# A loop of three turns in place of TensorE's unrolled attention steps, with one transpose added at two waits of each step

## The chip, the core and the metric

The kernel runs on one core of a Trainium2 chip. The metric is the device time of one execution in microseconds, lower is better; a median of several executions is given. Besides it there is a profile of one execution: for every engine the instructions with their start and duration. The engines are TensorE (PE in the profile; its weight loads are PEld, and what its sequencer does alone is PEldq), VectorE (DVE), ScalarE (ACT), GpSimd (POOL) and SyncE (SP), which here only issues the DMA transfers.

## What is computed

Attention over 2 x 8 heads, 576 positions and 64 channels, in two parts that are added; then a SiLU block and four weighted ReLU blocks over 1152 tokens of 512 channels.

```python
q_d = q.reshape(B, H, Sd, factor, D).mean(axis=3)      # factor 4; k_d and v_d likewise
out_up = np.repeat(sm_attn(q_d, k_d, v_d), factor, axis=2)
mask = np.abs(pos[:, None] - pos[None, :]) < factor
scores = np.where(mask, scale * q @ k.T, -1e9)
out_local = softmax(scores) @ v
x = (out_up + out_local), heads side by side           # 1152 x 512
h = x @ w_in;  x = (h * sigmoid(h)) @ w_out            # w_in 512 x 2048
out = sum over e of p[:, e] * (relu(x @ w1[e]) @ w2[e])   # 4 times 512 x 1024
```

## The kernel before

Every engine has a program of its own, written out by hand, and they meet at semaphores alone. There are N = 8 pairs of heads, and the attention is a pipeline over them. On TensorE step s does, in this order:

- scores(s): the mask as two matmuls against the identity, and 36 small score matmuls on top of it (lines 698 and 705 of the profile). They need the loaded q and k of pair s, and the bank back, which the normalised probabilities pl of pair s-1 tell.
- scores_down(s): four matmuls for the downsampled attention (line 718).
- turn_p0(s-1): four transposes of pl (line 659).
- values(s-2): 36 small matmuls with the transposed probabilities and a window of v (line 732), and the downsampled ones (line 739).
- turn_p1(s-1): the last transpose of pl and eight small ones of the downsampled probabilities pd (lines 659 and 664).

Each matmul in float32 is two matmuls and two weight loads in the profile, except transposes, which are one of each. So a step has 177 matmuls and 177 weight loads.

Meanwhile VectorE and ScalarE do the softmax of pair s in turn: VectorE the maximum and the subtraction, ScalarE the exponential, VectorE sum, reciprocal and product (line 559, which writes pl). ScalarE also copies what turn_p0(s-1) put into PSUM, and does so ahead of the exponential of pair s. GpSimd adds neighbouring positions for the downsampling, computes the low halves of x and of the first weight units. SyncE issues the loads of pair s+1 and the window of v for pair s-1.

Ahead of step 2 TensorE runs warm-up transposes of the identity in five groups (WARM; line 656): 12 ahead of all, 4 and 12 in step 0, 8 in step 1 between scores_down(1) and turn_p0(0), 5 ahead of scores(2). The steps are a Python loop, so TensorE's program has all of them one after another. In the last steps the first two tiles of layer one, in1(0, 0) and in1(0, 1) (line 753), are put between the transposes and values(7). From there on TensorE works through layer one and the four blocks of layer two (lines 753, 794, 810), in which it has hardware loops already: layer one's token blocks 1 and 2 are a loop of two turns (line 839), each with 16 tiles of 12 matmuls in and 12 out.

Of the kernel before, what the change touches and what calls it, by code (L numbers as in the profile page):

```python
# [14 lines left out]
P = 128  # L15
# [10 lines left out]
def program(nc, qk, vw, vr, w, probs, out, dims):  # L26
# [3 lines left out]
    SD = S // R  # L30
    HQ = SD // 2
# [26 lines left out]
    with ExitStack() as ctx:  # L58
# [3 lines left out]
        def sem(name):  # L62
            return ctx.enter_context(nc.semaphore(name))
# [9 lines left out]
        def asb(name, shape):  # L73
            return sb(name, shape, F32, att)
# [10 lines left out]
        ident = asb("ident", [P, P])  # L85
# [281 lines left out]
        def _(act):  # L367
            def copy(dst, src):
                return act.activation(dst, src, ACT.Copy)  # L369
# [52 lines left out]

            def evac_up(n):
                act.wait_ge(pv_done, n + 1)
                if n >= 1:
                    act.wait_ge(xf_done, n)
                copy(up[:, :].rearrange("p (a i q) -> p a i q", a=2, q=GQ // R),
                     ps[:, OUTB + 1, HC:HC + SD].rearrange("p (i a q) -> p a i q", a=2, q=GQ // R)).then_inc(up_done, 1)

            def x_high(n):  # L430
                act.wait_ge(xf_done, n + 1)
                copy(x_of(x_hi, n), xf[:, n, :]).then_inc(xhi_done, 1)

            def step(s):
# [71 lines left out]
        def _(dve):  # L506
            dve.memset(ident[:, :], 0.0).then_inc(zeroed, 1)
            dve.memset(band[:, :], 0.0).then_inc(zeroed, 1)
            dve.memset(pl[:, :, :, 0, W:HS], 0.0).then_inc(zeroed, 1)
            DSTEPS = 4  # L510

            def own(n, k):
                return n * DSTEPS + k

# [123 lines left out]
            with dve.Fori(0, E) as e:  # L638
                with dve.Fori(0, BLOCKS) as blk:
                    for f in range(FT2):  # L640
                        hidden2(e * (BLOCKS * FT2) + blk * FT2 + f, f)
                    for j in range(TT):
                        n = e * (BLOCKS * TT) + blk * TT + j
# [6 lines left out]
                            in1=o, op0=ALU.mult, op1=ALU.add).then_inc(out_done, 1)  # L650

        @block.tensor
        def _(pe):
            def warm(count):
                for _ in range(count):
                    pe.transpose(ps[:, OUTB, 0:P], ident[:, :], ident[:, :])  # L656

            def turn_local(n, bank, at, t):
                return pe.transpose(ps[0:PW, TB + bank, at:at + P],  # L659
                                    pl[:, n % 2, t, :, :].rearrange("p h j -> p (h j)")[:, 0:PW], ident[:, :])  # L660

            def turn_down(n, bank, at, i):
                s, h, half = i // 4, (i // 2) % 2, i % 2
                return pe.transpose(ps[0:HQ, TB + bank, at:at + HQ],  # L664
                                    pd[:, n % 2, 2 * h + half, s * HQ:(s + 1) * HQ], ident[0:HQ, 0:HQ])

            def turn_p0(n):
                pe.wait_ge(pl_ready, n + 1)
                if n == 0:
                    pe.wait_ge(zeroed, 3)  # L670
                if n >= 1:
                    pe.wait_ge(pd_out, n)
                for t in range(GT - 1):
                    ins = turn_local(n, 0, t * P, t)
                ins.then_inc(p0_turned, 1)

            def turn_p1(n):
                if n >= 1:
                    pe.wait_ge(p1_out, n)
                turn_local(n, 1, 0, GT - 1)  # L680
                pe.wait_ge(pd_ready, n + 1)
                for i in range(5):
                    ins = turn_down(n, 1, P + i * HQ, i)
                ins.then_inc(p1_turned, 1)
                pe.wait_ge(p0_out, n + 1)
                for i in range(3):
                    ins = turn_down(n, 0, i * HQ, 5 + i)
                ins.then_inc(pd_turned, 1)

            def scores(n):  # L690
                par = n % 2
                pe.wait_ge(qk_in[par], 16 * (n // 2 + 1))
                if n >= 1:
                    pe.wait_ge(pl_ready, n)
                else:
                    pe.wait_ge(mask_set, QP + 2)
                for h in range(2):
                    pe.matmul(ps[:, SLB + h, 0:LC], ident[:, :], mask[:, :, :].rearrange("p t j -> p (t j)"),  # L698
                              start=True, stop=False, skip_group_check=True)
                for g in range(G):  # L700
                    t, c = g // QP, g % QP
                    at = t * W
                    for h in range(2):
                        rows = slice(D * h, D * h + D)
                        ins = pe.matmul(ps[GQ * c:GQ * c + GQ, SLB + (h ^ g % 2), at:at + W],  # L705
                                        qk_raw[rows, par, GQ * g:GQ * g + GQ],
                                        qk_raw[rows, par, S + GQ * g:S + GQ * g + W], start=False, stop=True,
                                        skip_group_check=True)
                ins.then_inc(s_full, 1)

            def scores_down(n):
                pe.wait_ge(qkd_ready, 2 * n + 2)
                if n >= 1:
                    pe.wait_ge(pd_ready, n)
                for half in range(2):
                    for h in range(2):
                        rows = slice(D * h, D * h + D)
                        ins = pe.matmul(ps[0:HQ, SDB + h, half * SD:half * SD + SD],  # L718
                                        qd[rows, half * HQ:half * HQ + HQ], kd[rows, :], start=True, stop=True)
                ins.then_inc(sd_full, 1)  # L720

            def values(n):
                par = n % 2
                pe.wait_ge(p0_out, n + 1)
                pe.wait_ge(p1_out, n + 1)
                pe.wait_ge(vw_in[par], 32 * (n // 2 + 1))
                if n >= 1:
# [14 lines left out]
                ins.then_inc(pv_done, 1)  # L742
# [19 lines left out]
            def step(s):  # L762
                if s == N + 1:
                    in1(0, 1)
                if s == 2:
                    warm(WARM[4])
                stage(s, scores)
                if s == 0:
                    warm(WARM[1])
                stage(s, scores_down)  # L770
                if s < 2:
                    warm(WARM[2 + s])
                stage(s - 1, turn_p0)
                stage(s - 2, values)
                if s == N:
                    pe.wait_ge(xlo_done, XHALF)
                    pe.wait_ge(pd_ready, N)
                    in1(0, 0)
                stage(s - 1, turn_p1)
# [49 lines left out]
            pe.wait_ge(pl_ready, N)  # L829
            pe.wait_ge(pd_out, N)  # L830
            out1(0, 0)
            pe.wait_ge(xf_done, N)
            in1(0, 2)
            for f in range(3, FT1 + 2):
                if f < FT1:
# [49 lines left out]
```

## Time and profile before

| | |
|---|---|
| median of 3 executions | 680.59 us (678.07 to 682.2) |
| the profiled execution | 682.4 us, of it 680.5 from the first to the last instruction |
| TensorE busy | 665.4 us (98%), 4625 matmuls |
| VectorE, ScalarE, GpSimd busy | 156.5, 182.9, 164.6 us |
| instruction transfers of queue 8 | 21, 0.34 MB |
| mean granted TensorE clock | 0.976 of 2.4 GHz |

Busy TensorE means that a matmul is under way, at whatever clock. The clock that was granted is given as a share of 2.4 GHz: 1.00 is 2.4 GHz, 0.50 is 1.2. In the chain of waits "issue" is time in which the engine waited for nothing that the profile shows. Times in the rows are microseconds from the start of the span, those called mean, median or duration of one instruction nanoseconds.

### The profile page before, as it was taken

What the parts mean: (1) busy time and instruction counts of PE and PEld (TensorE: products, weight loads), DVE (VectorE), ACT (ScalarE), POOL (GpSimd) and SP (SyncE); (2) the same over time, 40 slices, a digit from 0 to 9 for tenths busy, and PEclk for the clock granted to TensorE, in tenths of its full rate; (3) what the DMA queues carried; (4) which work ended last, traced back from release to release, by engine and by line L of the source; (5) the groups of instructions that cost most, each with busy time, mean ns of one, the idle gap of its engine ahead of it and who ended that gap; (6) DMA issues with size and microseconds to landing.
All of it is one profiled execution on the core that took longest, in us unless ns stands there. A gap on an engine that the chain in (4) does not pass through costs nothing.

```text
span 680.5 us, 11829 instructions
## 1 busy us (share of the span) xinstructions
PE 665.4 (98%) x4625; PEld 616.8 (91%) x4625; DVE 156.5 (23%) x291; ACT 182.9 (27%) x385; POOL 164.6 (24%) x127
## 2 busy tenths in 40 slices
PE   7898999999999999999999999999999999999997
PEld 6676999999999999999898989898989898989996
DVE  5665311121112111212121212121212212121211
ACT  3555554332223244441111331010331010111010
POOL 4777476500000045561000460000550000000000
PEclk9786899999999999999999999999999999999999
DMA  8776124200000013331000140000220000000101
GB/s 262 180 196 142 59 110 153 95 1 1 1 0 1 0 67 124 118 129 57 0 0 0 63 155 31 0 0 0 92 92 0 0 0 0 0 31 16 46 0 46
DMA packets 11228, 38.59 MB, mean 57 GB/s; under 512 B 1536, under 2 KB 1536, under 8 KB 11200
## 3 DMA queue, kind: packets, MB, share of 16 engines
q1 hardware_dynamic: 11200, 38.19, 17.6%
q8 instruction: 21, 0.34, 0.2%
q14 instruction: 7, 0.06, 0.0%
HBM read 35.83 MB, written 2.36 MB: 56 GB/s over the span
## 4 chain that ended last, share of the span: by engine, by line
PE 97%; issue 1%; DVE 1%; ACT 0%; DVEq 0%; POOL 0%; POOLq 0%
PE ps L753 45%; PE ps L810 29%; PE ps L794 15%; PE ps L732 2%; PE ps L698 1%; PE ps L659 1%; PE ps L705 1%; PE ps L718 1%; PE ps L739 1%; PE ps L664 1%; PE ps L656 1%; DVE pl L559 0%; DVE ps L550 0%; DVE o_acc L647 0%; ACT plT L369 0%
## 5 line engine op out<-in xcount | busy, mean ns | idle before, releaser
L465 ACT ACTIVATE g_hi<-ps 128x384 fp32r<-128x384 f32 x96 | 47.2, 492 | 301.7 <-PE ps L753 301.7
L618 DVE SCALAR_TENSOR_TENSOR g_lo<-ps,g_hi 128x384 fp32r<-128x384 f32 x96 | 53.5, 557 | 270.5 <-ACT g_hi L465 270.5
L321 POOL TENSOR_TENSOR wa_lo<-w_raw,wa_hi 128x1024 f32 x20 | 47.9, 2401 | 215.4 <-ACT wa_hi L369 215.3
L753 PE MATMUL ps<-x_hi,wa_hi 128*128 (+1 forms) x288 | 97.6, 339 | 0.0
L753 PE MATMUL ps<-x_hi,wa_lo 128*128 (+1 forms) x288 | 97.4, 338 | 0.0
L753 PE MATMUL ps<-x_lo,wa_hi 128*128 (+1 forms) x288 | 97.2, 338 | 0.0
L753 PE MATMUL ps<-x_hi,wb_hi 128*128 (+1 forms) x288 | 96.9, 336 | 0.0
L753 PE MATMUL ps<-x_lo,wb_hi 128*128 (+1 forms) x288 | 96.9, 336 | 0.0
L753 PE MATMUL ps<-x_hi,wb_lo 128*128 (+1 forms) x288 | 96.8, 336 | 0.0
L321 POOL TENSOR_TENSOR wb_lo<-w_raw,wb_hi 128x1024 f32 x24 | 57.5, 2403 | 103.3 <-ACT wb_hi L369 103.0
L596 DVE TENSOR_TENSOR g_lo<-ps,g_hi 128x384 fp32r<-128x384 f32 x48 | 26.8, 557 | 155.1 <-ACT ps L460 155.1
L810 PE MATMUL ps<-wa_hi,g_lo 128*128 128x512 f32 x144 | 56.7, 394 | 0.0
L810 PE MATMUL ps<-wb_hi,g_lo 128*128 128x512 f32 x144 | 56.7, 394 | 0.0
L810 PE MATMUL ps<-wa_lo,g_hi 128*128 128x512 f32 x144 | 56.7, 394 | 0.0
L753 PEld LDWEIGHTS ps<-x_hi,wa_hi 128*128 128x128 f32 x288 | 54.6, 190 | 1.9 <-issue 0.4
L810 PE MATMUL ps<-wb_lo,g_hi 128*128 128x512 f32 x144 | 56.4, 391 | 0.0
L810 PE MATMUL ps<-wb_hi,g_hi 128*128 128x512 f32 x144 | 56.3, 391 | 0.0
L753 PEld LDWEIGHTS ps<-x_lo,wa_hi 128*128 128x128 f32 x288 | 54.6, 190 | 1.5
L810 PE MATMUL ps<-wa_hi,g_hi 128*128 128x512 f32 x144 | 56.0, 389 | 0.0
L753 PEld LDWEIGHTS ps<-x_lo,wb_hi 128*128 128x128 f32 x288 | 54.0, 188 | 1.6
L753 PEld LDWEIGHTS ps<-x_hi,wb_hi 128*128 128x128 f32 x288 | 54.0, 188 | 1.4
L753 PEld LDWEIGHTS ps<-x_hi,wa_lo 128*128 128x128 f32 x288 | 54.6, 190 | 0.0
(96 smaller groups left out, 923.5 us busy)
## 6 DMA issues: line engine op xcount, KB each, us to landing
w_raw<-w SPq DMA_DIRECT2D x48, 512.0 KB, 3.4
qk_raw<-qk SPq DMA_DIRECT2D x8, 579.0 KB, 5.9
v_win<-vw SPq DMA_DIRECT2D x16, 216.0 KB, 5.1
v_raw<-vr SPq DMA_DIRECT2D x8, 288.0 KB
out<-o_acc SPq DMA_DIRECT2D x9, 256.0 KB, 2.0
pr<-probs SPq DMA_DIRECT2D x1, 18.0 KB, 6.6
```

Of the source, the lines that this page charges most:

```text
L321: pool.tensor_tensor(lo[:, at, :].rearrange("p o n -> p (o n)"), w_raw[:, s, :], hi[:, at, :].rearrange("p o n -> p (o n)").bitcast(F32), ...
L465: act.activation(g_hi[:, f % GB, :], ps[:, HB + f % 4, 0:NB], ACT.Relu).then_inc(relu_done, 1)
L596: dve.tensor_tensor(g_lo[:, f % GB, :], ps[:, HB + f % 4, 0:NB], g_hi[:, f % GB, :].bitcast(F32), ALU.subtract).then_inc(g_ready, 1)
L618: dve.scalar_tensor_tensor(out=g_lo[:, f % GB, :], in0=ps[:, HB + f % 4, 0:NB], scalar=0.0, in1=g_hi[:, f % GB, :].bitcast(F32), op0=ALU.m ...
L656: pe.transpose(ps[:, OUTB, 0:P], ident[:, :], ident[:, :])
L659: return pe.transpose(ps[0:PW, TB + bank, at:at + P], pl[:, n % 2, t, :, :].rearrange("p h j -> p (h j)")[:, 0:PW], ident[:, :])
L664: return pe.transpose(ps[0:HQ, TB + bank, at:at + HQ], pd[:, n % 2, 2 * h + half, s * HQ:(s + 1) * HQ], ident[0:HQ, 0:HQ])
L698: pe.matmul(ps[:, SLB + h, 0:LC], ident[:, :], mask[:, :, :].rearrange("p t j -> p (t j)"), start=True, stop=False, skip_group_check=True)
L732: pe.matmul(ps[D * h:D * h + D, OUTB + g % 2, at:at + GQ], v_win[p0:p0 + W, par, g, :], plT[p0:p0 + W, par, t, GQ * c:GQ * c + GQ], start= ...
L753: ins = pe.matmul(dst, w[:, f % HALF, c], x[:, kt, at], start=(kt == 0 and i == 0), stop=(kt == KT - 1 and i == 2))
L794: ins = pe.matmul(ps[:, ACCB + j, 0:NB], w[:, f % HALF, c], g[:, f % GB, :], start=(f == 0 and i == 0), stop=(f == FT1 - 1 and i == 2))
L810: ins = pe.matmul(ps[:, ACCB + j, 0:DM], g[:, f % GB, c], w[:, f % HALF, KT * P:UNIT], start=(f == 0 and i == 0), stop=(f == FT2 - 1 and i ...
```

## The change

TensorE's steps 0 and 1 and what follows step 7 are written out; steps 2 to 7 become a loop (`pe.Fori`) of three turns over two steps. All addresses stay constants, since the two buffers alternate within a turn; the thresholds of the waits are computed from the loop's register. scores_down gets a transpose of the identity behind its waits, into columns of its own bank that nobody reads, and so does values. So that values(0) needs no case of its own, xf_done starts at one: VectorE sets a column of up to zero and raises it, and all waits on xf_done ask for one more. The eight warm-up transposes of step 1 come behind turn_p0(0), not ahead of it.

```diff
@@ scalar
             def evac_up(n):
                 act.wait_ge(pv_done, n + 1)
-                if n >= 1:
-                    act.wait_ge(xf_done, n)
+                act.wait_ge(xf_done, n + 1)
@@ vector
+            dve.memset(up[:, 0:1], 0.0).then_inc(xf_done, 1)
@@ tensor
-            def turn_p0(n):
+            def turn_p0(n, par):
                 pe.wait_ge(pl_ready, n + 1)
-                if n == 0:
+                if par == 0 and isinstance(n, int) and n == 0:
                     pe.wait_ge(zeroed, 3)
-                if n >= 1:
+                else:
                     pe.wait_ge(pd_out, n)
-            def scores(n):
-                par = n % 2
-                pe.wait_ge(qk_in[par], 16 * (n // 2 + 1))
-                if n >= 1:
+            def scores(n, par, turn):
+                pe.wait_ge(qk_in[par], 16 * turn + 16)
+                if not (isinstance(n, int) and n == 0):
                     pe.wait_ge(pl_ready, n)
             def scores_down(n):
-                pe.wait_ge(qkd_ready, 2 * n + 2)
-                if n >= 1:
+                pe.wait_ge(qkd_ready, n * 2 + 2)
+                if not (isinstance(n, int) and n == 0):
                     pe.wait_ge(pd_ready, n)
+                pe.transpose(ps[:, SDB + 1, 3 * SD - P:3 * SD], ident[:, :], ident[:, :])
-            def values(n):
-                par = n % 2
+            def values(n, par, turn):
                 pe.wait_ge(p0_out, n + 1)
                 pe.wait_ge(p1_out, n + 1)
-                pe.wait_ge(vw_in[par], 32 * (n // 2 + 1))
-                if n >= 1:
-                    pe.wait_ge(xf_done, n)
+                pe.wait_ge(vw_in[par], 32 * turn + 32)
+                pe.wait_ge(xf_done, n + 1)
+                pe.transpose(ps[:, OUTB, HC:HC + P], ident[:, :], ident[:, :])
-            for s in range(N + 2):
-                step(s)
+            scores(0, 0, 0)
+            warm(WARM[1])
+            scores_down(0)
+            warm(WARM[2])
+            scores(1, 1, 0)
+            scores_down(1)
+            turn_p0(0, 0)
+            warm(WARM[3])
+            turn_p1(0, 0)
+            warm(WARM[4])
+            with pe.Fori(1, N // 2) as i:
+                for par in range(2):
+                    s = i * 2 + par
+                    scores(s, par, i)
+                    scores_down(s)
+                    turn_p0(s - 1, 1 - par)
+                    values(s - 2, par, i - 1)
+                    turn_p1(s - 1, 1 - par)
+            turn_p0(N - 1, 1)
+            values(N - 2, 0, N // 2 - 1)
+            pe.wait_ge(xlo_done, XHALF)
+            pe.wait_ge(pd_ready, N)
+            in1(0, 0)
+            turn_p1(N - 1, 1)
+            in1(0, 1)
+            values(N - 1, 1, N // 2 - 1)
```

## Rows read from the trace of the kernel before

**Rows 1.** The chain that ended last: its shares of the span by engine
```profile
PE 97%; issue 1%; DVE 1%; ACT 0%; DVEq 0%; POOL 0%; POOLq 0%
```

**Rows 2.** The same chain in order of time: start us, us, what
```profile
24.50 2.37 issue
...
38.99 0.49 issue
...
49.53 0.47 issue
...
53.91 2.33 issue
```

**Rows 3.** Stretches: window us, PE busy (instructions), granted clock, DMA share, GB/s
```profile
27.10:37.30 10.20, 10.20 (x186) 0.50 0.78 183
...
40.70:44.10 3.40, 3.40 (x87) 0.50 0.47 123
44.10:57.80 13.70, 10.68 (x338) 1.00 0.66 164
57.80:74.80 17.00, 16.31 (x242) 0.50 0.44 102
```

**Rows 4.** One stretch, of PE, PEld, DVE, ACT, POOL busy (instructions), clock, DMA
```profile
26.87:38.99 12.12, 12.11 (x251) 9.61 (x251) 6.92 (x15) 5.21 (x19) 7.84 (x12) 0.58 0.81 204
```

**Rows 5.** DMA queues from 139 to 206.4 us (first row), from 206.4 to 273.5 (others)
```profile
q8 instruction: 4, 0.07, 0.4%
...
q1 hardware_dynamic: 1000, 3.65, 14.7%
q14 instruction: 1, 0.01, 0.0%
```

**Rows 6.** The second turn of layer one's loop, columns as in rows 4
```profile
206.40:273.50 67.10, 67.10 (x385) 67.10 (x385) 11.06 (x20) 25.16 (x44) 17.68 (x8) 1.00 0.15 55
```

**Rows 7.** Step 1: two rows of the chain, one of the timeline
```profile
12.79 1.02 PE ps L656 x8
...
14.78 0.49 ACT ps L409
...
12.77 0.56 DVE L536 TENSOR_TENSOR ps<-ps,mx 128x380 f32<-128x380 f32 x1
```

**Rows 8.** The chain at the low clock: four transposes of 128 columns
```profile
59.39 1.02 PE ps L659 x4
```

**Rows 9.** TensorE's sequencer by line: duration ns min/median/max, first and last start us
```profile
L747 PEldq EVENT_SEMAPHORE  x88: 51/51/51, 68.3 to 664.3; - x88
L747 PEldq ALU_OP  x42: 32/32/32, 141.2 to 647.7; - x42
L747 PEldq FUSED_REGOPS  x14: 42/125/136, 139.2 to 639.5; - x14
...
L839 PEldq COMPARE_BRANCH  x2: 76/159/242, 206.4 to 273.6; - x2
```

**Rows 10.** The chain: where scores of steps 5 to 7 and turn_p0(7) start
```profile
41.70 1.36 PE ps L698 x4
...
48.13 0.88 PE ps L698 x4
...
56.69 0.69 PE ps L698 x4
...
65.69 1.06 PE ps L659 x4
```

**Rows 11.** The chain: values(6) and values(7)
```profile
66.75 2.08 PE ps L732 x72
...
77.28 1.18 PE ps L732 x72
```

**Rows 12.** A stretch as in rows 4; the loads of v_win, from issue to landing
```profile
50.00:60.00 10.00, 7.66 (x218) 6.14 (x217) 6.62 (x14) 4.12 (x16) 9.69 (x13) 0.89 0.70 168
...
DMA to landing us min/median/max: 3.3/5.1/7.8
```

More of the change, by code:

```diff
@@ L430, in x_high @@
             def x_high(n):
-                act.wait_ge(xf_done, n + 1)
+                act.wait_ge(xf_done, n + 2)
                 copy(x_of(x_hi, n), xf[:, n, :]).then_inc(xhi_done, 1)
@@ L656, in warm, with turn_local, turn_down, turn_p1 @@
                     pe.transpose(ps[:, OUTB, 0:P], ident[:, :], ident[:, :])
-            def turn_local(n, bank, at, t):
+            def turn_local(par, bank, at, t):
                 return pe.transpose(ps[0:PW, TB + bank, at:at + P],
-                                    pl[:, n % 2, t, :, :].rearrange("p h j -> p (h j)")[:, 0:PW], ident[:, :])
-            def turn_down(n, bank, at, i):
+                                    pl[:, par, t, :, :].rearrange("p h j -> p (h j)")[:, 0:PW], ident[:, :])
+            def turn_down(par, bank, at, i):
                 s, h, half = i // 4, (i // 2) % 2, i % 2
                 return pe.transpose(ps[0:HQ, TB + bank, at:at + HQ],
-                                    pd[:, n % 2, 2 * h + half, s * HQ:(s + 1) * HQ], ident[0:HQ, 0:HQ])
-            def turn_p0(n):
+                                    pd[:, par, 2 * h + half, s * HQ:(s + 1) * HQ], ident[0:HQ, 0:HQ])
+            def turn_p0(n, par):
                 pe.wait_ge(pl_ready, n + 1)
-                if n == 0:
+                if par == 0 and isinstance(n, int) and n == 0:
                     pe.wait_ge(zeroed, 3)
-                if n >= 1:
+                else:
                     pe.wait_ge(pd_out, n)
                 for t in range(GT - 1):
-                    ins = turn_local(n, 0, t * P, t)
+                    ins = turn_local(par, 0, t * P, t)
                 ins.then_inc(p0_turned, 1)
-            def turn_p1(n):
-                if n >= 1:
+            def turn_p1(n, par):
+                if not (isinstance(n, int) and n == 0):
                     pe.wait_ge(p1_out, n)
-                turn_local(n, 1, 0, GT - 1)
+                turn_local(par, 1, 0, GT - 1)
                 pe.wait_ge(pd_ready, n + 1)
                 for i in range(5):
-                    ins = turn_down(n, 1, P + i * HQ, i)
+                    ins = turn_down(par, 1, P + i * HQ, i)
                 ins.then_inc(p1_turned, 1)
@@ L686, in turn_p1 @@
                 for i in range(3):
-                    ins = turn_down(n, 0, i * HQ, 5 + i)
+                    ins = turn_down(par, 0, i * HQ, 5 + i)
                 ins.then_inc(pd_turned, 1)
-            def scores(n):
-                par = n % 2
-                pe.wait_ge(qk_in[par], 16 * (n // 2 + 1))
-                if n >= 1:
+            def scores(n, par, turn):
+                pe.wait_ge(qk_in[par], 16 * turn + 16)
+                if not (isinstance(n, int) and n == 0):
                     pe.wait_ge(pl_ready, n)
@@ L711, in scores_down @@
             def scores_down(n):
-                pe.wait_ge(qkd_ready, 2 * n + 2)
-                if n >= 1:
+                pe.wait_ge(qkd_ready, n * 2 + 2)
+                if not (isinstance(n, int) and n == 0):
                     pe.wait_ge(pd_ready, n)
+                pe.transpose(ps[:, SDB + 1, 3 * SD - P:3 * SD], ident[:, :], ident[:, :])
                 for half in range(2):
@@ L720, in scores_down @@
                 ins.then_inc(sd_full, 1)
-            def values(n):
-                par = n % 2
+            def values(n, par, turn):
                 pe.wait_ge(p0_out, n + 1)
                 pe.wait_ge(p1_out, n + 1)
-                pe.wait_ge(vw_in[par], 32 * (n // 2 + 1))
-                if n >= 1:
-                    pe.wait_ge(xf_done, n)
+                pe.wait_ge(vw_in[par], 32 * turn + 32)
+                pe.wait_ge(xf_done, n + 1)
+                pe.transpose(ps[:, OUTB, HC:HC + P], ident[:, :], ident[:, :])
                 for g in range(G):
@@ L760, in _ @@
             WARM = (12, 4, 12, 8, 5)
[L762 to L779, printed above, removed]
             pe.wait_ge(ident_set, 1)
             warm(WARM[0])
-            for s in range(N + 2):
-                step(s)
+            scores(0, 0, 0)
[24 more added lines that the diff above has]
+            values(N - 1, 1, N // 2 - 1)
             def layer_out1(t, blk, f, w_hi, w_lo):
@@ L831, in _ @@
             out1(0, 0)
-            pe.wait_ge(xf_done, N)
+            pe.wait_ge(xf_done, N + 1)
             in1(0, 2)
```

## The prediction

> **What bounds the kernel now.** I read four views in this order. First the chain that ended last: 97% of it is TensorE work [rows 1], so what counts is where TensorE waits or runs slowly. Second, the same chain in order of time. After 79 us it has no wait in it worth naming; all that can be won lies in the attention steps ahead of that. There are four waits there that nothing in the profile releases ("issue"): 2.37, 0.49, 0.47 and 2.33 us [rows 2] (a fifth, shorter one lies in step 2). Third, the granted clock by stretch: it is at the low level (1.2 GHz) from 27.1 to 37.3, from 40.7 to 44.1 and from 57.8 to 74.8 us, and at the high one (2.4 GHz) between [rows 3]. Each fall comes within 4 us after one of the "issue" waits: 26.87 is followed by 27.1, 39.48 by 40.7, 56.24 by 57.8. The fifth wait, of 0.47 us at 49.53, and the softmax waits around 48 us did not bring the clock down.
>
> What are those waits? Between the end of the first at 26.87 and the start of the second at 38.99 TensorE executed 251 matmuls and 251 weight loads [rows 4]. With the sequencer's ten separate waits between them that is twice 256, and the other distances come out as once or twice 256 in the same way: the waits lie on a grid of 256 instructions. Instruction transfers of queue 8 are about 0.07 MB for 4, near 16 KB each, or 64 bytes an instruction [rows 5]. I take the waits for code that came late. Not every border costs something; those do which fall on a stretch with full data queues.
>
> **What a loop does to that.** The six looped steps hold eight such borders; as three turns over two steps only the first turn has to load code, if the blocks stay. The kernel before has a loop of this very size: layer one's loop over token blocks runs 385 matmuls and 385 loads a turn, as its second turn shows [rows 6]. An attention step has 177 matmuls and 177 loads, so a turn of two has 358 of each with the added transposes, slightly less. In the first turn of layer one's loop queue 8 fetched 4 blocks; in the second the transfers were those of queue 1 and one of queue 14, none of queue 8 [rows 5]. So a taken branch back over 770 instructions found its code in place.
>
> The Trainium skill says otherwise (Runtime: NRT & Kernel Launch, section Instruction fetch mechanics): only two blocks of 16 KB are kept, and a taken branch to a target outside them forces a fetch. By that rule each turn here would load again and the sum would be the second rival's, not mine. The rows of layer one's loop speak against it; but there long matmuls were queued over the branch, and at the end of an attention turn only short ones are, so the rule keeps a chance.
>
> **The sum**, against the profiled execution (span 680.5 us, 682.4 us in all; the median of the runs is 680.59, so this execution is 1.8 us slow). Everything is reckoned to the end of the last attention matmuls at about 79 us; after it TensorE is continuous, so what is won there is won at the end.
>
> 1. *Ahead of step 2.* The eight warm-up transposes of step 1 (1.02 us [rows 7]) move from ahead of turn_p0(0) to behind it. They stood on the path: turn_p0, its copy on ScalarE, then the exponential at 14.78 [rows 7]. Next late would be VectorE's subtraction, over at 13.33 [rows 7]. Gain 0.9 (bounds 0.5 and 1.02). Two added transposes, 0.13 us each (1.02/8), lie on the path: +0.26. Net -0.6.
> 2. *The other 14 transposes.* At the high clock 0.13 us [rows 7]; at the low one 0.26, by four 128-column transposes in 1.02 us [rows 8]. Step 2: 0.26. Steps 3 and 4, mostly low: 0.9. Steps 5 to 7: the one in scores_down delays turn_p0, its copy and the exponential, so 0.13 each; the one in values stands where TensorE has about 0.2 us to spare, I charge half. 0.6 in all. values(6) and values(7): 0.26. Sum +2.0 (bounds 0.9, if only those in scores_down count at the high clock, and 3.6, all 14 at the low price).
> 3. *Waits against registers.* A step has 15 waits in the Python code, whose thresholds are computed now. Known prices on TensorE's sequencer: 32 ns for an addition, 42 to 136 for a fused one, 51 for a separate wait [rows 9]; the step before had about six separate waits, 0.3 us. All 15 exposed at 51 ns would be 0.77; if they only replace the six, nothing or 0.3 less. Queued behind them are small matmuls, 72 of which pass in 1.18 us, 16 ns each [rows 11], so little work covers them as it does in layer one, except where TensorE waits for softmax anyhow. I take +0.15 a step, nearest to the 32 ns row with a third hidden: +0.9 for six (bounds -0.3 and +2.8).
> 4. *Back edges.* 242 ns at most for a taken branch, 76 for one not taken [rows 9]; two taken with a register move after each: +0.6.
> 5. *Late code in steps 4 to 7.* 0.49 + 0.47 + 2.33 = -3.3. The waits of steps 2 and 3 (a short one and 2.37) stay: that is the first turn, with the data queues as full as before (bounds: -5.7 if the 2.37 goes too, 0 if none goes).
> 6. *The clock.* With the long wait at 24.50 the first low stretch stays. The other two, by my reading, go, for steps 5 to 8 then have no code wait and a transpose more at either place. Scores start at 41.70, 48.13 and 56.69, and turn_p0(7) at 65.69 [rows 10]. The step from 48.13, all at the high clock, took 8.56 - 0.47 - 2.33 = 5.76 us. The step ahead of it took 6.43 and the one behind 9.00: -0.67 and -3.24. From 65.69 TensorE works without a gap to 74.85, 9.2 us at the low clock; the 72 small matmuls of values take 2.08 us low and 1.18 high [rows 11], the large ones half: -4.3. The end of step 4 gives 0.3. Sum -8.5 (bounds: 0, and -10.5 if part of the first low stretch goes as well).
> 7. *Next late.* GpSimd is busy 9.69 of 10 us from 50 to 60 [rows 12], and the window load of pair 6 is issued behind its work and takes 3.3 to 7.8 us to land [rows 12]; values(6) would want it about 5 us sooner than before. I charge 0.3. Layer one's weights are no bound: their copies are issued by ScalarE behind the last attention steps and move with them.
>
> Initialising up, and counting xf_done from one instead of testing n, costs nothing: one more small VectorE memset at the start, while the first load is on its way. It would cost under 0.1 us without that cover. The columns that the added transposes write are read by nobody, and their waits are those that the steps had.
>
> -0.6 + 2.0 + 0.9 + 0.6 - 3.3 - 8.5 + 0.3 = -8.6, so 682.4 - 8.6 = **673.8 us**.
>
> **Rivals.**
> - *The clock does not hold.* The fall at 40.7 came after only 0.49 us of waiting, in a stretch of small matmuls; the 0.3 us of a back edge and the waits on registers may do as much. Then term 6 shrinks to between 0 and half, and transposes cost the low price: -0.6 + 2.6 + 0.9 + 0.6 - 3.3 = +0.2 at the one end, about -4 at the other: 678 to 682.6. For it: the clock fell three times in 48 us. Against it: 13.7 us at the high level from 44.1, a whole step without an added transpose in it [rows 3].
> - *Slower: the branch loads its code again.* At each of the two back edges the target is gone, and the whole latency shows, as in the wait of 2.37 us [rows 2]; the straight-line waits stay, and so do the low stretches. Sum: -0.6 + 2.6 + 0.9 + 0.6 + 2 x 2.4 = +8.3, about 690.7. It decides as soon as a turn is larger than what is kept. Against it: layer one's second turn [rows 5, 6].
> - *The loop does not do what it is for.* Code comes late elsewhere (at the end of the first turn, on leaving the loop), in the same total, and the clock falls as before: -0.6 + 2.6 + 0.9 + 0.6 = +3.5 less what little moves, 683 to 686.
>
> **How the numbers follow.** Forecast with the clock held: 0.58 (its own range 670.5 to 677.0; the terms with bounds of several us are 2, 3 and the first low stretch). Clock not held: 0.22. Loop without effect: 0.09. Code loaded again: 0.11. A measurement of this kernel can tell about 0.5%, 3.4 us. Faster than 677.2: the 0.58 and nearly half of the second case, 0.68. Within: the rest of it and most of the third, 0.19. Slower: 0.13. The range leaves out some 0.08 below and 0.12 above: 670.0 to 683.5.
>
> **What would show it.** Right: instruction transfers of queue 8 fall from 21 to about 15; no "issue" wait of over 0.4 us on TensorE between 35 and 75 us; granted clock high from some 38 us on; scores 6.1 us apart in steps 5 to 7; the last values over at 70 to 71 us. Wrong: queue 8 keeps its count, or a wait of over 2 us directly behind a taken branch of the new loop (second rival); clock low after 45 us with no code wait ahead of it (first rival). Steps over 6.6 us apart at the high clock would say that term 3 is too small. The prediction would also be wrong if the wait at 24.50 vanished or grew with the shift of the 256-instruction grid, by up to 3 us either way.

## The result, and the profile after

The changed kernel takes 677.91 us (median of 20 executions, 676.58 to 679.45) and the kernel before, in the same number, 680.75 (677.27 to 685.54). The ratio is 0.9949, with a 95% interval of 0.9931 to 0.9966: 0.5% faster by the ratio, 2.8 us between the medians, where 8.6 were forecast. The profiled execution of after took 677.18 us, 675.2 of it from first to last instruction; that of before 682.4 and 680.5. So the two profiles differ by 5.3 us. The medians differ by less because the profiled execution of before was slower than most (1.7 us over its median) and that of after faster (0.7 us under).

The page of after, the answer to the table of before: the granted clock in 40 slices, and the transfers of instructions.

```profile
PEclk9888999999999999999999999999999999999999
...
q8 instruction: 15, 0.25, 0.1%
```

From 31 to 60 us (the second and third turn and the first 3 us behind them) the DMA queues of after show no instruction transfer of queue 8 at all (before had six from 26 to 60 us):

```profile
q1 hardware_dynamic: 1424, 5.22, 72.5%
q14 instruction: 2, 0.02, 0.1%
```

So the loop fetched no code after its first turn, as layer one's does [rows 5]. The loop's branches cost TensorE's sequencer what the ones of layer one cost [rows 9]:

```profile
L773 PEldq COMPARE_BRANCH  x3: 76/212/243, 30.8 to 57.2; - x3
```

What TensorE waited for from 30 to 75 us in after (line waited with, who released it, us in total, times, longest). Of the waits of [rows 2] the one of the first turn is left, at 24.29 us (third line, from the chain), and the three behind it are gone; but a new one has come, for the window load:

```profile
PE ps L727 <- DMA v_win<-vw: 1.5, 1, 1.5
PE ps L659 <- ACT pdT L369: 1.0, 1, 1.0
...
24.29 2.26 issue
```

The timeline of after: scores of pairs 5 to 7, then turn_p0(7) and the transpose that opens values(6), with the idle time ahead of them in brackets. These answer to [rows 10] and [rows 11].

```profile
40.94 0.91 PE L697 MATMUL ps<-mask,ident 128*128 128x190 f32 x4
...
46.80 0.91 PE L697 MATMUL ps<-mask,ident 128*128 128x190 f32 x4
...
52.68 0.91 PE L697 MATMUL ps<-mask,ident 128*128 128x190 f32 x4
...
59.52 0.62 PE L659 MATMUL ps<-ident,pl 128*102 128x128 f32 x4 [0.96 <-ACT pdT L369]
61.61 0.30 PE L727 MATMUL ps<-ident 128*128 128x128 f32 x1 [1.48 <-DMA v_win<-vw]
```

The steps are 5.9 us apart. turn_p0(7) starts 6.2 us sooner than before; then part of it is lost again. SyncE's timeline shows why: the window loads of pair 6 are issued from 56.03 us on, behind the v load of pair 7 at 55.68, which had waited for GpSimd. The window load of the chain took until 61.37. The last two lines are the same two issues in before: they came only 1.2 us sooner in after.

```profile
55.68 0.31 SPq L213 DMA_DIRECT2D v_raw<-vr  x1
56.03 2.59 SPq L220 DMA_DIRECT2D v_win<-vw  x4
...
56.41 4.95 DMA v_win<-vw
...
56.91 0.31 SPq L213 DMA_DIRECT2D v_raw<-vr  x1
57.27 7.20 SPq L220 DMA_DIRECT2D v_win<-vw  x4
```

And the clock, in windows of TensorE alone (us, busy, instructions, granted clock, DMA share, GB/s), answering to [rows 3]:

```profile
28.00:38.20 10.20, 10.20 (x183) 0.50 0.77 200
38.30:62.10 23.80, 21.31 (x649) 1.00 0.73 181
62.20:68.90 6.70, 6.70 (x84) 0.50 0.21 61
```

It held from 38 to 62 us, and fell behind the 0.96 and 1.48 us of waiting. values(6) and layer one's first tile ran at the low clock and took 7.2 us (first three lines, from the chain); values(7) and the second tile, the same work at the high one, took 4.0:

```profile
61.91 1.88 PE ps L731 x72
63.79 1.16 PE ps L738 x8
64.95 4.14 PE ps L752 x12
...
69.69 2.16 PE ps L752 x12
71.86 0.11 PE ps L727
71.96 1.18 PE ps L731 x72
73.14 0.64 PE ps L738 x8
```

### The profile page after: what moved, and what is told of

The parts are those of the page before. It is cut to its first block, busy times and chain, and to the rows that moved or that the text cites. A ratio compares the mean times of both kernels' runs of the same rounds, so it can differ in the third digit from the quotient of the medians.

```text
span 675.2 us, 11883 instructions
## 1 busy us (share of the span) xinstructions
PE 662.9 (98%) x4641; PEld 614.8 (91%) x4641; DVE 156.4 (23%) x292; ACT 182.3 (27%) x385; POOL 164.3 (24%) x127
## 4 chain that ended last, share of the span: by engine, by line
PE 95%; POOL 2%; issue 1%; DMA 1%; DVE 1%; ACT 0%; SPq 0%; DVEq 0%; POOLq 0%
PE ps L752 45%; PE ps L814 29%; PE ps L798 15%; PE ps L731 1%; PE ps L697 1%; PE ps L704 1%; DMA v_win<-vw 1%; PE ps L718 1%; PE ps L738 1%; PE ps L659 1%; PE ps L656 1%; POOL v L285 0%; PE ps L664 0%; POOL wa_lo L328 0%; PE ps L714 0%
```

## The experiments

The expectations name theories. A: the gain is the code that no longer comes late, with the clock that holds behind it, and the missing part is the late window load (A2: and any other wait of 1 us). B: the transposes carry the gain. C: nothing was missing, the profile of before was a slow one. D: the clock falls for reasons of its own. E: work of the full array in the steps holds it.

Below, "low time" of an execution is 2 x (1 - its mean granted clock) x its span, in us; for a run its median over the executions. Runs of one group share a chip and the executions of before; after has 20 executions of before of its own, on a chip that isn't known. The edits are told against the kernel named, and shown without the lines between them; the interval is that of the ratio to before. The median of before moves from 679.3 to 682.0 us between groups, so medians of different groups compare only to about 2 us; the conclusions rest on pairs of one group where there are such. A run has 5 to 12 executions, which mostly spread over 2 to 8 us, so within a group, too, a difference of under 2 us is within the noise.

| run | kernel | median us | ratio, 95% interval | low time us |
|---|---|---|---|---|
| | before, with after | 680.75 | | not known |
| | after | 677.91 | 0.9949 (0.9931 to 0.9966) | 21.6 |
| | before, with e1 to e4 | 679.98 | | 24.5 |
| e1 | after, no transposes | 677.78 | 0.9959 (0.9935 to 0.9983) | 22.3 |
| e2 | before + transposes | 681.65 | 1.0033 (1.0012 to 1.0053) | 24.5 |
| e3 | before, warm-up moved | 679.61 | 0.9994 (0.9969 to 1.0019) | 27.1 |
| e4 | after, window load first | 674.23 | 0.9927 (0.9897 to 0.9957) | 15.5 |
| | before, with e5 to e8 | 679.82 | | 27.1 |
| e5 | after, both orders | 673.87 | 0.9897 (0.9865 to 0.9930) | 11.4 |
| e6 | before, both orders | 675.15 | 0.9923 (0.9892 to 0.9953) | 14.8 |
| e7 | e5, no transposes | 673.41 | 0.9886 (0.9849 to 0.9923) | 16.1 |
| e8 | after, split later | 676.05 | 0.9929 (0.9904 to 0.9954) | 17.5 |
| | before, with e9 to e11 | 681.97 | | 28.6 |
| e9 | e5, gap filled | 672.59 | 0.9870 (0.9841 to 0.9899) | 12.0 |
| e10 | e7, gap filled | 675.29 | 0.9909 (0.9882 to 0.9936) | 20.2 |
| e11 | e5, three transposes | 671.34 | 0.9849 (0.9819 to 0.9879) | 7.4 |
| | before, with e12 to e15 | 679.31 | | 24.4 |
| e12 | after, three transposes | 679.56 | 0.9997 (0.9977 to 1.0017) | 21.0 |
| e13 | e11 unrolled | 678.11 | 0.9979 (0.9957 to 1.0001) | 12.8 |
| e14 | e5, five transposes | 671.74 | 0.9918 (0.9887 to 0.9950) | 2.0 |
| e15 | e11, unit 1 later | 672.12 | 0.9892 (0.9870 to 0.9914) | 7.4 |
| | before, with e16 to e18 | 681.37 | | 27.2 |
| e16 | e11, copy later | 670.58 | 0.9845 (0.9812 to 0.9878) | 4.0 |
| e17 | e5, copy later | 670.12 | 0.9835 (0.9802 to 0.9868) | 6.7 |
| e18 | e17 unrolled | 677.03 | 0.9938 (0.9915 to 0.9961) | 13.5 |

**The parts of the change, one by one.** e1 is the loop without its transposes; values opens with an 8-column matmul that carries the wait.

```diff
             def scores_down(n):
-                pe.transpose(ps[:, SDB + 1, 3 * SD - P:3 * SD], ident[:, :], ident[:, :])
             def values(n, par, turn):
-                pe.transpose(ps[:, OUTB, HC:HC + P], ident[:, :], ident[:, :])
+                pe.matmul(ps[:, OUTB, HC:HC + 8], ident[:, :], ident[:, 0:8], start=True, stop=True)
```

> The changed kernel without its two added transposes; values begins with an 8-column matmul of the identity instead, which carries the wait. Theory A (the gain is the late code that is gone and the clock that then holds): instruction transfers stay at 15, no wait of TensorE for code after the first turn, steps 5 to 7 about 0.3 us shorter each than the changed kernel's 5.88 us; if the clock holds without transposes 676 to 677.5 us, if it falls in one step more 678 to 680. Rival B (the transposes carry the gain by holding the clock): the low clock comes back in steps 4 to 7 as in the kernel before, 680 to 682 us.

677.78 us, 22.3 us of low time: the changed kernel's time without its transposes, so rival B is out. Its profile had 15 instruction transfers, a first-turn wait of 4.16 us and the wait for the window load of 1.93 us; steps 5 to 7 came 5.7 us apart. As the kernel stands, the loop carries the gain, and the transposes neither add nor take more than these runs can tell.

e2 is the reverse, the two transposes in the unrolled kernel.

```diff
             def scores_down(n):
+                pe.transpose(ps[:, SDB + 1, 3 * SD - P:3 * SD], ident[:, :], ident[:, :])
             def values(n):
+                pe.transpose(ps[:, OUTB, HC:HC + P], ident[:, :], ident[:, :])
```

> The kernel before, unrolled, with the two transposes of each step added and nothing else. Theory A: 21 instruction transfers, the waits for code stay and stand where 256 instructions are over, that is earlier in the work than before; transposes cost 14 to 16 times 0.13 to 0.26 us on the path: 681.5 to 684 us. Rival B: the clock holds by them alone and the kernel takes 677 to 679 us.

681.65 us, 0.33% slower than before, as theory A had it. There are waits for code again (3.9 us in this profile, 5.9 in that of before), and they moved in the work while they kept their count of instructions: matmuls, weight loads and sequencer's instructions of TensorE ahead of them are 961, 1473 and 2241 in e2's trace, and 705, 961, 1473, 1985 and 2241 in that of before, all 256 or a multiple of it apart. The last one, which stood in turn_p1 (line 664) in before, stands in values here (line 741 of e2, the downsampled matmuls). TensorE's longer waits for code in e2:

```profile
PE ps L705 <- issue: 2.2, 1, 2.2
PE ps L741 <- issue: 1.3, 1, 1.3
```

e3 moves the eight warm-up transposes alone.

```diff
                 if s < 2:
-                    warm(WARM[2 + s])
+                if s == 0:
+                    warm(WARM[2])
                 stage(s - 1, turn_p0)
+                if s == 1:
+                    warm(WARM[3])
```

> The kernel before with only the eight warm-up transposes of step 1 put behind turn_p0(0). By the prediction's term 1 the scores of pair 2 start 0.9 us sooner: 679.6 to 680.2 us. In the changed kernel they started only 0.2 us sooner, beside two added transposes ahead of them; if the first low clock or a load takes the gain back, no difference: 680.7 us.

Scores of pair 2 start at 16.11 us in its chain, 0.9 us sooner than the 17.04 of the chain of before, as term 1 said.

```profile
16.11 0.88 PE ps L698 x4
```

But the time is 0.9994 of before, with an interval that holds both no change and the 0.9 us (0.13%). It isn't settled whether the gain reaches the end.

**Where the missing part was.** e4 changes only SyncE's order in the changed kernel.

```diff
                 stage(s + 1, load_qk)
-                stage(s, load_v)
                 stage(s - 1, load_win)
+                stage(s, load_v)
```

> The changed kernel with SyncE issuing the window load of a step ahead of the v load of that step. Theory A (the missing part of the gain is values(6) waiting 1.5 us for its window load, issued at 56.0 us behind a v load that waits for GpSimd, and the low clock of 6.8 us behind it): the load is issued at about 52 us, the wait is gone, the clock stays high from 38 us on, 673.5 to 675.5 us, 2.5 to 4.5 below the changed kernel. Rival C (the missing part never was there, the profiled execution of before was a slow one; something else, GpSimd or the softmax of pair 7, is as late): 677 to 678 us.

674.23 us, 3.7 below the changed kernel and 3.6 below e1 on its own chip: theory A. The ten executions spread from 671.4 to 680.4 us; by their means the two differences are 2.9 and 2.7, so the size is known to about 2 us. The wait for the window load is gone. What came in its place is GpSimd: scores_down waits for kd, the downsampled k, 2.05 us in step 7, since GpSimd's split of weight unit 2 (the low halves of a block of layer one's weights, 2.8 us) stood ahead of it. The clock fell once more in this profile, for some 6.7 us from 57.3 us on, just behind turn_p0(7) and its wait of 0.96 us for ScalarE.

```profile
PE ps L714 <- POOL kd L310: 2.9, 2, 2.1
```

e5 moves that split, too, from GpSimd's step 5 to its step 8; e8 moves the split alone, with SyncE's order as it was.

```diff
+        LATER = {1: 0, 2: 1, N - 1: 2, N: 3}
-                if s - 1 in EARLY:
-                    low_quarters(EARLY[s - 1])
+                if s - 1 in LATER:
+                    low_quarters(LATER[s - 1])
```

> As the run with the window load first, and besides GpSimd splits weight unit 2 (four quarters, 2.8 us) in its step 8, not in step 5. Theory A (with the window load early, GpSimd is the next late: scores_down(7) waited 2.05 us for kd, and the clock fell behind that): no wait of TensorE for GpSimd in step 7, the clock high until layer one, 671 to 672.5 us. Rival C (the clock falls for want of work anyhow, or the split is late for layer one): 674 us or more.

> The changed kernel with unit 2 split in GpSimd's step 8 and SyncE's order as it was. Theory A: the v load of pair 7 waits for GpSimd's vd(5), which comes 2.8 us sooner, so the window load of pair 6 is issued at about 53 us, not 56, and lands at about 58.5: the wait before values(6) goes here too, 673.5 to 675.5 us. Rival C (order of the loads alone matters): 677 to 678 us.

e5 gave 673.87 us and e8 676.05. Both took their wait away. e8 did better than rival C and a little worse than theory A: a second, independent way of taking the window load's wait away gains some 2 us over after. e5 was little better than e4, against my 671 to 672.5. One reason shows in ScalarE's waits from 30 to 46 us, here of e8: its copy of weight unit 2 (the high halves) waits for the load, and behind that copy stand the copies that turn_p0(3) needs. TensorE waited 2.95 us there in e8, 0.8 in e5.

```profile
ACT wa_hi L370 <- DMA w_raw<-w: 3.0, 1, 3.0
```

The other shows in e5's clock. It has no wait for the window load, and still the clock falls where it fell in after, around the 0.97 us that turn_p0(7) waits for ScalarE (first line), and stays low for 10.1 us (second line: window, busy, granted clock, DMA share, GB/s). In e1, which has both waits, the clock is low already between them (the last three lines):

```profile
55.52 1.06 PE L660 MATMUL ps<-ident,pl 128*102 128x128 f32 x4 [0.97 <-ACT pdT L370]
55.40:65.50 10.10, 9.98 (x107) 0.50 0.30 85
...
59.37 1.07 PE L659 MATMUL ps<-ident,pl 128*102 128x128 f32 x4 [0.95 <-ACT pdT L369]
59.30:60.50 1.20, 1.07 (x4) 0.50 1.02 207
62.37 0.57 PE L726 MATMUL ps<-ident 128*128 128x8 f32 x2 [1.93 <-DMA v_win<-vw]
```

So the window load's wait isn't needed for this fall. In after the low stretch begins only behind both waits, and which of them brought it on isn't shown.

**The loop's worth at other orders, first attempt.** e6 is the kernel before with both orders changed; e7 is e5 without transposes (edits as above).

> The kernel before, unrolled and without added transposes, with both orders changed (window load ahead of the v load, unit 2 split in GpSimd's step 8). Tells what the loop is worth where nothing else is late. Theory A: the waits for code stay (5.6 us in the profile of before) and the clock falls behind them: 677 to 679.5 us, 5 to 8 above the loop with the same orders. Rival B (the orders do it, the loop is worth no more than before): 673 to 675 us.

> The loop without added transposes (8 columns in values to carry the wait) with both orders changed. Theory A (transposes only cost; the clock falls behind waits of microseconds, not for want of them): 0.5 to 2 us below the same kernel with transposes, 669.5 to 671.5 us. Rival B (transposes hold the clock): a low stretch in steps 5 to 7 without a wait of over 1 us ahead of it, 673 to 676 us.

e6 took 675.15 us: neither theory A's 677 to 679.5 nor B's 675 at most, just outside it. So the two orders gain 4.7 us without any loop. Part of that is that code came less late: e6's profile has 2.4 us of waits for code, that of before 5.9. Against e7 (673.41) the loop would be worth 1.7 us, but with six executions each that is within the noise. e7 missed theory A's 669.5 to 671.5 and came out where rival B had it (673 to 676), though not by B's sign: its low stretch of 10.2 us from 38.5 us on begins behind a wait of 1.22 us. e7 and e5 are the same within their spread, with 16.1 and 11.4 us of low time.

**What holds the clock.** e9 and e10 put five transposes of the identity into the last wait, ahead of turn_p0(7).

```diff
+            pe.wait_ge(xf_done, N - 1)
+            warm(5)
             turn_p0(N - 1, 1)
```

> As e5 (loop, transposes, both orders) with five transposes of the identity ahead of turn_p0(7), behind a wait for final(5), where TensorE otherwise has 0.97 us of nothing. Theory A2 (waits of about 1 us are enough to bring the clock down, and what the change lacks is that any one of them is left): no low stretch of 7 to 10 us over values(6) and layer one's first tile in most executions, median low time under 8 us, 671 to 672.5 us. Rival D (a fall comes every so often for a reason that the waits don't explain): low time and time as e5, 673.9 us.

> As e7 (loop without added transposes, both orders) with the same five ahead of turn_p0(7). Theory A2: low time and time fall below e7's 673.4 us, to 670.5 to 672 us. If transposes in the steps do hold the clock, it stays above e9.

e9's low time is e5's (12.0 against 11.4), and e10's is above e7's (20.2 against 16.1). The added wait, for VectorE's final(5), was 1.76 us in e9's profile and 1.74 in e10's, longer than the gap that it should fill. So the fill did not fill, and the pair says nothing on whether a single wait of 1 us decides. But it does say something on the transposes in the steps, by which alone the two differ: with them 672.59 us, without 675.29, on one chip, and all six executions of e10 but one lie above the slowest of e9. Here one transpose at each place gains 2.7 us.

e11 put three transposes at either place of the steps where e5 has one, e14 five, and e12 three in the changed kernel as it is:

```diff
-                pe.transpose(...)
+                pe.transpose(...)
+                pe.transpose(...)
+                pe.transpose(...)
```

> As e5 with three transposes instead of one at either place of each step. Price by the changed kernel's rows: the transpose in scores_down takes 0.26 us of the path at the high clock, further ones 0.13, so 16 times 2 x 0.13 less what stands in spare time, +3 to +4 us: 677 to 678 us. If work of the full array holds the clock, low time falls under e5's 11 us and the time rises by less, 674 to 676 us.

> The changed kernel with three transposes instead of one at either place, orders as they were. If full-array work holds the clock (theory E): low time falls from 21.6 us to under 15 and the time to 675 to 676.5 us, although the 32 transposes more take 4 us of TensorE. If only waits matter (theory A): the window-load wait stays, low time stays near 20 us, 679 to 681 us.

> As e11 with five transposes at either place. Theory E with a bound: low time is nearly gone already at three (7 us), so two more at each place only cost, 0.13 us each, 32 of them, some of it in spare time: 673 to 675.5 us. If they still pay: 670 to 671 us.

e11 took 671.34 us, under both of its forecasts; e12 (679.56) came out as theory A had it and e14 (671.74) between its two. This speaks against the part of theory A by which transposes only cost. With both orders changed and 0, 1, 3, 5 transposes at each place the low time is 16.1, 11.4, 7.4, 2.0 us and the ratio 0.989, 0.990, 0.985, 0.992 (the last two on chips of their own). The low time falls with each step; in time the 64 transposes that e14 has more than e5 come back almost wholly, where they alone would take some 8 us of TensorE (64 times 0.13). No run put as much work of small matmuls in their place, so it isn't shown that it matters that they use the full array. The profile of e14 is at the high clock from 6.9 to 669 us (two of its six executions, with 12 us of low time, took 677), and these are all of TensorE's waits from 16 us on:

```profile
PE ps L660 <- ACT pdT L370: 0.9, 1, 0.9
PE ps L698 <- DVE pl L560: 0.7, 1, 0.7
```

In the changed kernel as it is, e12, they hold nothing and take back the gain: no faster than before, low time 21.0. The wait for the window load (1.27 us in its profile) and the fall at that place stay.

e13 unrolls e11; e15 has GpSimd split weight unit 1 a step later, too.

```diff
-        LATER = {1: 0, 2: 1, N - 1: 2, N: 3}
+        LATER = {1: 0, 3: 1, N - 1: 2, N: 3}
```

> The kernel before, unrolled, with three transposes at either place and both orders changed: e11 without the loop (and with the warm-up where it was). The waits for code come at every 256th instruction, now nearer to each other in the work. If the loop is worth its waits for code (3 to 5 us a run): 674 to 677 us. If the clock was all: the time of e11's kind, 671 to 673 us.

> As e11, and GpSimd splits weight unit 1 in its step 4, not in step 3. In e11's profile scores_down(4) waited 0.5 us for kd and turn_p0(3) 1.6 us behind it, and the clock fell at 39.8 for 10 us. If those waits bring it down: low time near 0 to 5 us, 669.5 to 671 us. If not: as e11, 671.3 us.

e13 took 678.11 us, over the 674 to 677 forecast, and 6.0 over e15 beside it on the same chip (from which it also differs by GpSimd's step for unit 1 and by the place of the warm-up). Its executions run from 672.8 to 681.1 us, and the profiled one, which had 1.3 us of waits for code, was the fastest. e15 itself was no better than e11 (672.12 against 671.34): it made the load of unit 2 later still, and turn_p0(3) waited 2.69 us. That pointed to ScalarE's copy.

**What is left when that is out of the way.** e16 and e17 are e11 and e5 with ScalarE's copy of weight unit 2 in step 5.

```diff
+        SPLIT = {1: 0, 2: 1, 5: 2, N: 3}
-                if s in EARLY:
-                    split_hi(EARLY[s])
+                if s in SPLIT:
+                    split_hi(SPLIT[s])
```

> As e11 (loop, three transposes, both orders), and ScalarE copies weight unit 2 in its step 5, not in step 4. If that copy's wait for its load holds up the chain: no wait before turn_p0(3), low time near 0 to 4 us, 669.5 to 671 us. If not: 671 to 672 us with the low stretch at 40 us.

> As e5 (loop, one transpose, both orders) with the same later copy. If waits alone decide the clock: as low in low time as e16, and by the transposes saved some 2 us faster, 668 to 670 us. If full-array work decides too: a low stretch stays in most executions, 671 to 673 us.

> As e17 with TensorE's steps written out as in the kernel before (warm-up behind turn_p0(0) as in the loop). It differs from e17 by the loop alone. The waits for code return at every 256th instruction: 3 to 6 us more than e17, 674 to 677 us. If the loop is worth only its 3.3 us of waits less its own overhead: 672 to 674 us.

670.58 and 670.12 us: the fastest of all, 1.6% under the kernel before, and e17 is the changed kernel with three orders changed and nothing else. The wait before turn_p0(3) is gone in both. Three transposes leave a little less low time than one (4.0 against 6.7), and no less time: theory A and theory E are both right in part.

e18 is e17 with TensorE's steps written out. On the same chip, beside e17's 670.12, it took 677.03 us. TensorE's waits from 5 to 75 us, first in e17:

```profile
PE ps L699 <- DVE pl L561: 1.7, 2, 1.0
PE ps L733 <- issue: 1.2, 1, 1.2
PE ps L661 <- ACT pdT L371: 1.0, 1, 1.0
PE ps L729 <- DVE xf L582: 0.3, 1, 0.3
```

and the ones of e18 up to 80 us that e17 has not, or has shorter:

```profile
PE ps L743 <- issue: 3.0, 1, 3.0
PE ps L707 <- issue: 2.0, 3, 0.8
...
PE ps L732 <- ACT plT L371: 0.8, 1, 0.8
PE ps L736 <- issue: 0.3, 1, 0.3
```

5.4 us of waits for code against 1.2 in the profiles, and 13.5 us of low time against 6.7 in the runs. So with the three orders changed and the transposes in place the loop alone is worth 6.9 us; in the changed kernel as it is, loop, transposes and moved warm-up together are worth 2.8. The 6.9 us are not the loop's gain over the best unrolled kernel, though: e18 is no faster than e6 (ratios 0.9938 and 0.9923), which is unrolled, too, and has neither the transposes nor the moved copy. Against e6, on another chip, e17 gains about 0.9%, some 6 us, of which part may be the copy's. The unrolled kernel with the moved copy and no transposes was not run.

## Why the prediction was wrong

Its direction was right, and so was the mechanism that it named for the gain. Its size was not: the measured gain, 2.8 us, is a third of the forecast, and 677.9 lies in the range given for all cases (670.0 to 683.5) and outside that of the forecast case. The step that failed is term 7, the window load, charged at 0.3 us where the wait was 1.5 and its removal gained some 3 to 4, and with it the half of term 6 that lay behind the loop, where the clock fell again. Another 2.4 us are the luck of the two profiled executions: the sum was set against a slow one of before. By its own steps, in the two profiles:

*Code.* Right: 15 transfers, none in turns two and three, the waits of steps 4 to 7 gone and the first turn's left. The rival by which a taken branch loads its code again is refuted by the profile of after. That the waits lie on a grid of 256 instructions held in e2, where they moved in the work and not in the count.

*Term 1.* The moved warm-up gave 0.9 us, as said (e3's start of step 2). The transposes beside it were mis-sized a little. The one in scores_down(1) takes 0.26 us of the chain at the high clock, not 0.13: I had taken the distance of transposes in a row, and this one stands behind small matmuls. The one in scores_down(0), behind warm-up transposes, takes 0.11.

```profile
6.82 0.93 PE ps L656 x4
7.76 0.11 PE ps L714
...
12.62 0.26 PE ps L714
```

Step 2 began 0.2 us sooner in after, not 0.6. The two transposes explain 0.1 of that; 0.3 lies in the four warm-up transposes of step 0, which took 0.93 us here and 0.59 in before, and also in e2 and e17, which have the same transpose behind them.

*Terms 2 to 4.* Oversized together, by some 2 us. Steps 5 to 7 came 5.9 us apart, where 5.76 were measured before and 6.1 forecast. Branches, waits against registers and transposes cost 0.1 us a step in sum, though a single transpose takes up to 0.26. It may be that the thresholds are computed while TensorE waits for softmax anyway; no run tests that. By the sum's terms up to there turn_p0(7) would have started at 65.7 - 4.9 = 60.8 us; it started at 59.5. This was luck for the total: up to here the change did better than forecast, by 1.3 us.

*Term 7, the step that failed first.* I saw that the window load of pair 6 was issued behind GpSimd's work and took 3.3 to 7.8 us to land [rows 12], and charged 0.3 us. I had let the issue move with the steps. It moved by 1.2 us, from 57.27 to 56.03, while turn_p0(7) moved by 6.2: it hangs on GpSimd, which was busy for 10.7 of the 11 us ahead of it and did not get faster. Issue at 56.0 and 5 us to land should have been set against a values(6) wanted at about 60. The wait was 1.5 us, not 0.3. Taking it away was worth 3.7 us in e4 by the medians, 2.9 by the means; what is more than the wait goes with the low time, which fell from 21.6 to 15.5 us.

*Term 6, the largest.* Between the two profiles its first half came: the 6.2 us at turn_p0(7) hold it. (Of the 3.24 us counted for the last step ahead of turn_p0(7) 2.2 came, 9.00 against 6.84 us; it ends in the wait of 0.96 us.) Its second half, the 4.3 us behind turn_p0(7), did not come. From there to the end of values(7) before took 13.4 us; the sum has 3.8 less for after, that is 9.6, and it took 14.3. The missing 4.7 are the wait of 1.5 and 3.2 of low clock, 7.2 us for work that takes 4.0 at the high one. Which of the two waits there brought the clock down stays open (e1, e5).

Between the medians there was less to win from the start. The profiled execution of before was at the low clock for longer than most: 33 us, against a median of 24 to 29 in the groups. The low time of after, 21.6 us, is some 3 to 7 us less than those, where the forecast reckoned with about 10 left. And over whole executions the time follows low time less steeply than I took: over the 47 executions of before of the first two groups it rises 0.24 us with each microsecond of low time (a correlation, not an experiment); I had taken 8.5 us for the 20.4 of the two later stretches [rows 3], or 0.42. For the dense stretch behind turn_p0(7) that price was right: 3.2 of 7.2 us is 0.44. The rival "the clock does not hold", at 678 to 682.6 with a chance of 0.22, was the one nearest, though not for its reason: the clock held through the back edges and fell only after the loop, where TensorE waited for ScalarE and for a load.

*Medians.* The sum was put against one execution and given as a forecast for the median. 1.7 us of it was that execution's own.

What stays open: what exactly makes the clock fall. It fell behind waits of 1 to 3 us in most profiles, and work in the steps (e11, e14) made that rarer, yet e5 and e7 differ by 5 us of low time and not in their median, while e9 and e10, which differ in the same way, are 2.7 us apart. Nor was the wait in the first turn tried by itself.

## What to carry to other kernels

Look for waits that nothing releases on an engine with much straight code, and count instructions between them. If the count is a multiple of one number (here 256), suspect code that comes late; here a hardware loop took those waits away from its second turn on. Before giving an engine its microseconds back, set every load and every copy that it will want sooner against what issues it: a load behind another engine's wait does not move. Price a state that varies between executions (here the clock) by many executions, never by one profile. And find the worth of an edit against the best kernel without it, not only against the same kernel with the edit taken out.

## What the runs showed that I had not expected

The wait for code in the first turn (step 3) was 2.2 to 4.2 us in the profiles of before, after, e1, e2 and e3, 1.5 and 0.9 in e12 and e8, and between nothing and 1.2 us in all those with the window load issued first, where the data transfers stand in another order at that moment. That the order does it was not tried by itself. Transposes in a stretch of small matmuls can come almost for nothing: e14 spends 80 where e7 has none, and the ratios to before are 0.992 and 0.989. One at each place did nothing in after (e1) and between e5 and e7, and gained 2.7 us between e9 and e10. And an edit has no worth of its own: taking the loop away cost 1.7 us, within the noise, with both orders and no transposes (e6), and 6.9 with the transposes and the moved copy (e18).
